# Attention inside a feed-forward kernel: the 144 keys of a pair of heads laid out key by key, as 128 and 16 rows

## The chip, the core and the metric

The kernel runs on one core of one Trainium2 chip. A core has TensorE (PE, with its weight loads shown as an engine of their own, PEld), VectorE (DVE), ScalarE (ACT), GpSimd (POOL) and the DMA queues, of which this kernel uses SyncE's (SP). The metric is the device time of one execution in microseconds; less is better. Each engine works through its own list of instructions in order and waits on semaphores for the others.

## What is computed

An attention over pooled keys and values, then two feed-forward layers:

```python
k_p = k.reshape(B, H, Sp, pool, D).mean(axis=3)      # B 8, H 8, S 576, D 64, pool 8, Sp 72
v_p = v.reshape(B, H, Sp, pool, D).mean(axis=3)
scores = scale * np.matmul(q, k_p.transpose(0, 1, 3, 2))
scores = scores - np.max(scores, axis=-1, keepdims=True)
attn = np.exp(scores)
attn = attn / (np.sum(attn, axis=-1, keepdims=True) + 1e-09)
out = np.matmul(attn, v_p)                            # then (4608 tokens, 512)
x = leaky(x @ w1_in) @ w1_out                         # 512 -> 2048 -> 512
x = (h * clip(h + 3, 0, 6) / 6) @ w2_out, h = x @ w2_in
```

All is float32. Where the kernel wants float32 accuracy at the rate of the shorter format, it splits an operand into a rounded part (`_hi`) and the rest (`_lo`) and adds three products: hi by hi, hi by lo, lo by hi.

## The kernel before

**Units and tiles.** The attention is cut into 32 units: 8 batches by 4 pairs of heads. A unit has 576 queries, 72 pooled keys for each of its two heads, and 64 columns of values for each. The feed-forward work is cut into 9 tiles of 512 tokens for each layer, 18 in all, each of 8 steps. The four units of batch 0 run ahead of everything; the 28 units of batches 1 to 7 are laid between the products of tiles 0 to 6, four units to a tile. That stretch is 45 to 735 us of the span; behind it only feed-forward work stands.

**What sets the order.** It is written by hand. A tile has 64 places (8 steps by 8), and `UNIT_PLACES` (line 49) says at which place of the tile each of the nine stages of each of its four units stands, on every engine alike: (0, 3, 4, 5, 6, 9, 11, 12, 14) for the first unit, and so on. TensorE's list is feed-forward products with a stage's products put in at its place. What an engine does at a place, it does there, late or not.

**The stages of a unit** (`stage`, once for each engine; ps_att is its two PSUM banks, 0 and 1):

- `place_k`: ACT puts the summed keys of both heads into `kT`, 144 columns, head 0 in 0 to 71 and head 1 in 72 to 143. `scores`: PE makes 5 products (L1910), one for each block of 128 queries. The blocks begin at 0, 128, 256 (half 0) and at 384, 448 (half 1), so that the last one shares 64 queries with the one before it. DVE takes the maxima (L1538) and subtracts them (L1543) for the two halves. `exp` is ACT's (L1193); `normalize` and `divide` are DVE's (L1549, L1553, L1557). `prob` then holds 10 rows of 72 for each query: block by block, head by head.
- `turn_p0`, `turn_p1`: PE turns the probabilities (L1928) so that keys stand on the partitions. A piece is one head of one block: 72 keys by 128 queries. Head 0 goes to bank 0, head 1 to bank 1. Half 0 has 6 whole pieces. Half 1 has 4, and those of the last block turn only its new 64 queries (`AGAIN`), that is 64 of its 128 rows. ACT rounds both heads at once into `pT_hi` (L1202), DVE subtracts for `pT_lo` (L1564).
- `pv0`, `pv1`: PE multiplies with the values, for each head the three products v_hi by pT_hi, v_hi by pT_lo, v_lo by pT_hi (L1729 to L1731): 72 rows, 384 queries in `pv0` and 192 in `pv1`, six products each. `v_hi[:, hd]` is zero but for its head's 64 columns, so that all six add into one bank. ACT copies the result (L1211).

**The values** come as 72 rows for each head; DVE sums them over the pool of 8 (`sum_v`, L1577), ACT rounds them (`round_v`, L1220), POOL subtracts (`v_lo`, L847). They go to their own places of the tile, some 7 places or more ahead of `pv0` in all tiles but tile 0.

**Batch 0** uses plain float32 values and probabilities (`v_f`, `pT_f`, L1942), two products where the others have six.

## Time and profile before

| | |
|---|---|
| median of 3 runs | 1659.18 us (1653.12 to 1662.17) |
| profiled execution | 1650.04 us, of which the span is 1648.2 us |
| PE busy, matmuls | 1636.8 us, 99%, 13947 instructions |
| PEld busy, weight loads | 1614.8 us, 98% |
| DVE, ACT, POOL busy | 68%, 41%, 26% |
| stretch with attention, 45 to 735 us | 5735 matmul records, PE busy 686.7 of 690 us |
| granted TensorE clock | 0.999 of 2.4 GHz |

Matmul records overlap: each lasts some 0.28 us from its first to its last cycle, while the next begins some 0.11 us after it. So what an instruction costs TensorE is read from the distance between the starts of two records, not from its length. A stage put between feed-forward products costs the distance from its first record to a product behind it, less what the products themselves take.

### The profile page before, as it was taken

Reading aid. Unit: us, or ns where it says so; the run is one execution under the profiler, and the core shown is the slowest. Engines: PE = TensorE matmul, PEld = TensorE weight load, DVE = VectorE, ACT = ScalarE, POOL = GpSimd, SP = SyncE. Lnnn points to the kernel's source line nnn. Section 1 sums busy time; section 2 is a strip of 40 time slices with the busy share of each in tenths; the row PEclk is TensorE's granted clock in tenths of the full one; section 3 lists DMA queues with packets and bytes.
Section 4 is the critical chain, followed back from the end, with each engine's and each line's share of the span. In section 5 each row is a group of like instructions: output and inputs, shape, how many; then the busy total and the mean of one; then the engine's idle time right before and its main releaser. Section 6 shows DMA issues by size and latency. Waiting matters only on the chain.

```text
span 1648.2 us, 40178 instructions
## 1 busy us (share of the span) xinstructions
PE 1636.8 (99%) x13947; PEld 1614.8 (98%) x13947; DVE 1120.2 (68%) x2159; ACT 676.4 (41%) x1427; POOL 429.3 (26%) x451
## 2 busy tenths in 40 slices
PE   9999999999999999999999999999999999999998
PEld 8999999999999999999999999999999999999998
DVE  6768777686776867756455666676767676766665
ACT  5554443333332433333233444444444444444443
POOL 4346552021120212103335572030211111111100
PEclk9999999999999999999999999999999999999999
DMA  7746878778686786867789998898989898989894
GB/s 222 259 140 221 284 254 261 225 216 277 201 268 219 231 267 201 272 193 262 260 254 358 312 358 302 297 337 296 341 297 336 282 339 294 336 288 340 294 323 156
DMA packets 228572, 447.94 MB, mean 272 GB/s; under 512 B 23872, under 2 KB 48448, under 8 KB 219200
## 3 DMA queue, kind: packets, MB, share of 16 engines
q1 hardware_dynamic: 228416, 445.74, 80.9%
q8 instruction: 113, 1.85, 0.4%
q14 instruction: 43, 0.35, 0.1%
HBM read 379.58 MB, written 66.06 MB: 270 GB/s over the span
## 4 chain that ended last, share of the span: by engine, by line
PE 81%; DVE 2%; issue 1%; DMA 1%; ACT 0%; POOL 0%; DVEq 0%; ACTq 0%
PE ps_h L1804 36%; PE ps_y L1750 31%; PE ps_y L1891 5%; PE ps_att L1891 4%; PE ps_att L1928 2%; PE ps_att L1910 2%; PE ps_att L1729 1%; PE ps_att L1731 1%; PE ps_att L1730 1%; DMA w_in_split<-stage 1%; POOL stage L934 0%; DVE prob L1557 0%; PE ps_att L1741 0%; DVE h L1458 0%; DVE gate L1392 0%
## 5 line engine op out<-in xcount | busy, mean ns | idle before, releaser
L1804 PE MATMUL ps_h<-xs_hi,ring 128*128 128x256 f32 x3808 | 796.0, 280 | 1.8 <-DVE h L1458 0.8
L1804 PEld LDWEIGHTS ps_h<-xs_hi,ring 128*128 128x128 f32 x3808 | 635.9, 188 | 6.8 <-issue 3.6
L1804 PE MATMUL ps_h<-xs_lo,ring 128*128 128x256 f32 x1904 | 528.1, 277 | 0.0
L1804 PEld LDWEIGHTS ps_h<-xs_lo,ring 128*128 128x128 f32 x1904 | 358.6, 188 | 0.0
L1138 ACT ACTIVATE g_hi<-gate 128x512 fp32r<-128x512 f32 x288 | 182.1, 632 | 380.2 <-DVE gate L1392 200.6
L1750 PE MATMUL ps_y<-g_hi,wout_hi 128*128 128x256 f32 x1152 | 320.2, 278 | 0.6 <-DVE y_stage L1454 0.6
L1750 PE MATMUL ps_y<-g_hi,wout_lo 128*128 128x256 f32 x1152 | 319.2, 277 | 0.0
L1750 PE MATMUL ps_y<-g_lo,wout_hi 128*128 128x256 f32 x1152 | 319.1, 277 | 0.0
L1750 PEld LDWEIGHTS ps_y<-g_hi,wout_hi 128*128 128x128 f32 x1152 | 216.3, 188 | 1.2 <-DVE y_stage L1454 1.0
L1750 PEld LDWEIGHTS ps_y<-g_lo,wout_hi 128*128 128x128 f32 x1152 | 217.1, 188 | 0.0
L1750 PEld LDWEIGHTS ps_y<-g_hi,wout_lo 128*128 128x128 f32 x1152 | 216.3, 188 | 0.0
L1458 DVE TENSOR_TENSOR u<-ps_h,p 128x256 f32<-128x256 f32 x272 | 114.1, 419 | 124.0 <-PE ps_h L1804 104.7
L1127 ACT ACTIVATE pre<-h,three 128x512 f32<-128x512 f32 x144 | 103.2, 716 | 206.2 <-DVE h L1458 179.7
L1750 PE MATMUL ps_y<-wout_hi,g_hi 128*128 128x256 f32 x640 | 177.1, 277 | 0.0
L1750 PE MATMUL ps_y<-wout_lo,g_hi 128*128 128x256 f32 x640 | 177.1, 277 | 0.0
L1750 PE MATMUL ps_y<-wout_hi,g_lo 128*128 128x256 f32 x640 | 177.1, 277 | 0.0
L1398 DVE SCALAR_TENSOR_TENSOR gate<-pre,h 128x512 f32<-128x512 f32 x144 | 107.1, 744 | 67.2 <-ACT pre L1127 67.2
L1458 DVE TENSOR_TENSOR h<-ps_h,u 128x256 f32<-128x256 f32 x272 | 113.7, 418 | 54.6 <-PE ps_h L1804 53.0
L1407 DVE TENSOR_TENSOR g_lo<-gate,g_hi 128x512 fp32r<-128x512 f32 x144 | 109.8, 763 | 56.8 <-ACT g_hi L1138 56.6
L1411 DVE SCALAR_TENSOR_TENSOR g_lo<-gate,g_hi 128x512 fp32r<-128x512 f32 x144 | 105.6, 734 | 35.0 <-ACT g_hi L1138 34.9
L913 POOL TENSOR_TENSOR xs_lo<-x_stage,xs_hi 128x512 fp32r<-128x512 f32 x20 | 28.7, 1434 | 386.7 <-ACT xs_hi L1107 386.7
L1750 PEld LDWEIGHTS ps_y<-wout_lo,g_hi 128*128 128x128 f32 x640 | 120.3, 188 | 0.0
(155 smaller groups left out, 2862.1 us busy)
## 6 DMA issues: line engine op xcount, KB each, us to landing
ring<-w_in_split SPq DMA_DIRECT2D x920, 256.0 KB, 4.0
w_sums<-w_out_sums SPq DMA_DIRECT2D x64, 1024.0 KB, 6.2
w_in_split<-ring SPq DMA_DIRECT2D x56, 256.0 KB, 3.7
w_in_split<-stage SPq DMA_DIRECT2D x56, 256.0 KB, 3.9
k_raw<-in_kT SPq DMA_DIRECT2D x32, 288.0 KB, 4.0
q_raw<-in_qT SPq DMA_DIRECT2D x32, 288.0 KB, 5.3
v_raw<-in_v SPq DMA_DIRECT2D x32, 288.0 KB
x0T<-x_stage SPq DMA_DIRECT2D x32, 288.0 KB, 4.2
```

Of the source, the lines that this page charges most:

```text
L913: nc.gpsimd.tensor_tensor(xs_lo[second][:, r], x_block(r), xs_hi[second][:, r].bitcast(F32), ALU.subtract).then_inc(x_ready, 1 if r < NT4 ...
L1127: nc.scalar.activation(pre[:, upper], h[:, upper], ACT.Relu, bias=three[:]).then_inc(pre_ready, 1)
L1138: nc.scalar.activation(g_hi[layer == 2][:, g_slot(i, upper)], gate[:, upper], ACT.Copy, scale=1.0 / 6.0 if layer == 2 else 1.0).then_inc(g ...
L1398: nc.vector.scalar_tensor_tensor(gate[:, upper], pre[:, upper], 6.0, h[:, upper], ALU.min, ALU.mult).then_inc(gate_ready, 1)
L1407: nc.vector.tensor_tensor(g_lo[0][:, slot], gate[:, upper], g_hi[0][:, slot].bitcast(F32), ALU.subtract).then_inc(g_ready, 1)
L1411: nc.vector.scalar_tensor_tensor(g_lo[1][:, slot], gate[:, upper], 1.0 / 6.0, g_hi[1][:, slot].bitcast(F32), ALU.mult, ALU.subtract).then_ ...
L1458: return nc.vector.tensor_tensor(to, banks[bank], other, ALU.add)
L1750: mm = pe.matmul(bank[:, cols], left[a], right[b][:, cols], start=first and half == 0 and n == 0, stop=last and n == 2, skip_group_check=True)
L1804: mm = pe.matmul(banks[BANK_OF[r]], a, b[:, r, c, :], start=r in OPENS and c == 0 and n == 0, stop=c == 1 and n == 2, skip_group_check=True)
L1891: mm = pe.matmul(pair_banks[r], left[a], right[b], start=i == 0 and n == 0 and r in PAIR_OPENS, stop=i == HF - 1 and n == 2, skip_group_ch ...
L1910: mm = pe.matmul(u.ps[:, half, at * PAIR_KEYS:(at + 1) * PAIR_KEYS], q_of(b, c)[:, begins:begins + P], u.kT[:], start=True, stop=True)
L1928: mm = pe.transpose(at.ps[0:KEYS, hd, to:to + P - rows.start], u.prob[rows, SLOTS[half].start + 2 * j + hd, :], ident[rows, rows])
```

## The change

The 144 scores of a block stand key by key: key 0 of head 0, key 0 of head 1, key 1 of head 0. Keys 0 to 63 of both heads are then 128 adjacent columns, and keys 64 to 71 are 16.

- `place_k` writes every other column of `kT`. The maxima, sums, subtraction and division read and write `prob` as block, key, head (a step of two elements between the keys of one head).
- `turn_p0`, `turn_p1`: for each block one piece of 128 keys and one of 16, over all 128 queries; the last block, too, is turned whole. The 16-row pieces of half `half` go to bank `half` and come first, the 128-row pieces to the other bank. Batch 0 keeps 72-row pieces, one for each head, and turns its last block whole.
- ACT makes three copies for each half: the 16 rows and the 128 rows of `pT_hi`, and once more the 16 rows to partitions 64 to 79. DVE makes two subtractions: that of the 16 rows goes to partitions 32 to 47 of the same buffer, that of the 128 rows to `pT_lo`.
- `pv0`, `pv1`: four products: v_hi by p_hi, v_lo by p_hi (128 rows), one over 80 rows that does all three products of the last 16 rows at once (its weights hold v_hi, v_hi and v_lo at partitions 0, 32 and 64), and v_hi by p_lo (128 rows). They wait separately for what each needs.
- The values are loaded as 128 rows, and as 96 rows that repeat the last 16 six times, 256 KB and 192 KB instead of 288 KB, in two DMAs. `sum_v` sums 128 partitions and then multiplies by a mask (`v_masked`, new), which clears the other head's columns. `round_v` is one instruction of 256 columns, `v_lo` one of 128 rows and one of 16. The mask is made once by DVE (`make_mask`), and POOL clears `pT_hi` once when the products of batch 0 are done.

The tables of places are unchanged. In the built program the turns of 16 rows name a tile of 128 by 32 of the array, all others 128 by 128; before, the turns of 64 queries named 64 by 128, all others 128 by 128.

The diff, cut to its core:

```diff
...
+FULL = 64
+REST = 2 * (KEYS - FULL)
+REST_LO = slice(32, 32 + REST)
+AGAIN = slice(64, 64 + REST)
+VALUE_COPIES = 6
+VALUE_ROWS = VALUE_COPIES * REST
...
-                sp.dma_start(buffers(b, c).v_raw[:], v[b, c]).then_inc(v_loaded[c], 16)
+                to = buffers(b, c).v_raw
+                if first(b):
+                    sp.dma_start(to[0:KEYS], v_first[c]).then_inc(v_loaded[c], 16)
+                else:
+                    sp.dma_start(to[:, 0], v_full[b - 1, c]).then_inc(v_loaded[c], 16)
+                    sp.dma_start(to[0:VALUE_ROWS, 1], v_rest[b - 1, c]).then_inc(v_loaded[c], 16)
...
+            pool.wait_ge(pv_done, 2 * PAIRS)
+            pool.memset(units[0].pT_hi[0:AGAIN.stop].bitcast(F32), 0.0).then_inc(pT_zeroed, 1)
             blocks_lo(2)
             v_lo(1, 0)
...
+                        for rows, bank in ((slice(0, REST), half), (slice(0, P), 1 - half)):
+                            nc.scalar.activation(u.pT_hi[rows, bank, 0:n_q], u.ps[rows, bank, 0:n_q],
+                                                 ACT.Copy).then_inc(pT_hi_ready, 1)
+                        act.wait_ge(pT_hi_ready, 3 * (2 * n + half) + 1)
+                        nc.scalar.activation(u.pT_hi[AGAIN, half, 0:n_q],
+                                             u.pT_hi[0:REST, half, 0:n_q].bitcast(F32), ACT.Copy
+                                             ).then_inc(pT_hi_ready, 1)
...
-                for hd in range(2):
-                    nc.scalar.activation(u.v_hi[:, hd, hd * D:(hd + 1) * D], u.v_sum[:, hd, :],
-                                         ACT.Copy).then_inc(v_hi_ready, 1)
+                nc.scalar.activation(u.v_hi[:], u.v_masked[:].rearrange("p s h d -> p s (h d)"),
+                                     ACT.Copy).then_inc(v_hi_ready, 1)
...
-                    nc.vector.tensor_tensor(u.pT_lo[:, :, 0:n_q], u.ps[0:KEYS, :, 0:n_q],
-                                            u.pT_hi[:, :, 0:n_q].bitcast(F32), ALU.subtract
-                                            ).then_inc(pT_ready, 1)
+                    for k, (to, rows, bank) in enumerate((
+                            (u.pT_hi[REST_LO, half], slice(0, REST), half),
+                            (u.pT_lo, slice(0, P), 1 - half))):
+                        dve.wait_ge(pT_hi_ready, 3 * (2 * n + half) + k + 1)
+                        nc.vector.tensor_tensor(to[:, 0:n_q], u.ps[rows, bank, 0:n_q],
+                                                u.pT_hi[rows, bank, 0:n_q].bitcast(F32),
+                                                ALU.subtract).then_inc(pT_ready, 1)
...
+                dve.wait_ge(v_summed, n + 1)
+                nc.vector.tensor_tensor(u.v_masked[:],
+                                        u.v_sum[:].unsqueeze(2).to_broadcast([P, 2, 2, D]),
+                                        u.v_mask[:].unsqueeze(3).to_broadcast([P, 2, 2, D]),
+                                        ALU.mult).then_inc(v_masked, 1)
...
-                            rows = slice(AGAIN if begins == S - P else 0, P)
-                            to = begins + rows.start - PART_BEGINS[half]
-                            mm = pe.transpose(
-                                at.ps[0:KEYS, hd, to:to + P - rows.start],
-                                u.prob[rows, SLOTS[half].start + 2 * j + hd, :],
-                                ident[rows, rows])
+                            to = begins - PART_BEGINS[half]
+                            row = u.prob[:, BLOCKS_AT[half].start + j]
+                            if first(b):
+                                rows, keys = KEYS, row[:, :, bank]
+                            else:
+                                part = slice(FULL, KEYS) if bank == half else slice(0, FULL)
+                                rows, keys = ((P, REST)[bank == half],
+                                              row[:, part].rearrange("p k h -> p (k h)"))
+                            mm = pe.transpose(at.ps[0:rows, bank, to:to + P], keys, ident[:])
...
-                        pe.wait_ge(pT_ready, 2 * n + half + 1)
-                        for hd in range(2):
-                            mm = product(u.ps[:, half, 0:n_q],
-                                         (u.v_hi[:, hd, :], u.v_lo[:, hd, :]),
-                                         (u.pT_hi[:, hd, 0:n_q], u.pT_lo[:, hd, 0:n_q]),
-                                         hd == 0, hd == 1)
+                        acc, p_hi = u.ps[:, half, 0:n_q], u.pT_hi[:, 1 - half, 0:n_q]
+                        pe.wait_ge(pT_hi_ready, 3 * (2 * n + half) + 2)
+                        pe.wait_ge(pT_ready, 2 * (2 * n + half) + 1)
+                        pe.matmul(acc, u.v_hi[:, 0], p_hi, start=True, stop=False)
+                        pe.matmul(acc, u.v_lo[:], p_hi, start=False, stop=False)
+
+                        pe.wait_ge(pT_hi_ready, 3 * (2 * n + half) + 3)
+                        pe.matmul(acc, u.v_hi[0:AGAIN.stop, 1], u.pT_hi[0:AGAIN.stop, half, 0:n_q],
+                                  start=False, stop=False)
+                        pe.wait_ge(pT_ready, 2 * (2 * n + half) + 2)
+                        mm = pe.matmul(acc, u.v_hi[:, 0], u.pT_lo[:, 0:n_q], start=False, stop=True)
```

**TensorE's list**, before, at the second turn of a unit and with its neighbours (L1804 and L1750 are feed-forward products; the shape is that of the result):

```order
L1750 MATMUL ps_y<-g_hi,wout_lo 128x256
L1928 MATMUL ps_att<-ident,prob 72x128
L1928 MATMUL ps_att<-ident,prob 72x64
L1928 MATMUL ps_att<-ident,prob 72x128
L1928 MATMUL ps_att<-ident,prob 72x64
L1804 MATMUL ps_h<-xs_hi,ring 128x256
L1804 MATMUL ps_h<-xs_lo,ring 128x256
```

The same place after (L1829 and L1883 are the feed-forward products now):

```order
L1829 MATMUL ps_y<-g_hi,wout_lo 128x256
L2013 MATMUL ps_att<-ident,prob 16x128 x2
L2013 MATMUL ps_att<-ident,prob 128x128 x2
L1883 MATMUL ps_h<-xs_hi,ring 128x256
L1883 MATMUL ps_h<-xs_lo,ring 128x256
```

Two short and two long turns took the place of an alternation of whole and half blocks; nothing else moved. The first turn has six pieces of 72 rows before, and three of 16 and three of 128 after.

**VectorE's list**, before, from the second subtraction of one unit to the sum of the next unit's values:

```order
L1564 TENSOR_TENSOR pT_lo<-ps_att,pT_hi 72x2x192
L1458 TENSOR_TENSOR u<-ps_h,p 128x256
L1458 TENSOR_TENSOR h<-ps_h,u 128x256
L1458 TENSOR_TENSOR h<-ps_h,p 128x256
L1392 SCALAR_TENSOR_TENSOR gate<-h 128x512
L1571 TENSOR_REDUCE k_sum<-k_raw 128x72
L1458 TENSOR_TENSOR h<-ps_h,u 128x256
L1577 TENSOR_REDUCE v_sum<-v_raw 72x128
L1407 TENSOR_TENSOR g_lo<-gate,g_hi 128x512
```

The same place after:

```order
L1620 TENSOR_TENSOR pT_hi<-ps_att,pT_hi 16x192
L1620 TENSOR_TENSOR pT_lo<-ps_att,pT_hi 128x192
L1506 TENSOR_TENSOR u<-ps_h,p 128x256
L1506 TENSOR_TENSOR h<-ps_h,u 128x256
L1506 TENSOR_TENSOR h<-ps_h,p 128x256
L1440 SCALAR_TENSOR_TENSOR gate<-h 128x512
L1627 TENSOR_REDUCE k_sum<-k_raw 128x72
L1506 TENSOR_TENSOR h<-ps_h,u 128x256
L1648 TENSOR_REDUCE v_sum<-v_raw 128x128
L1651 TENSOR_TENSOR v_masked<-v_sum,v_mask 128x256
L1455 TENSOR_TENSOR g_lo<-gate,g_hi 128x512
```

One subtraction became two, and the multiplication by the mask stands between the sum of the values and the subtraction for g_lo.

**ScalarE's list** in tile 0, around the first turn of the first unit of batch 1, before:

```order
L1138 ACTIVATE g_hi<-gate 128x512
L1202 ACTIVATE pT_hi<-ps_att 72x768
L1220 ACTIVATE v_hi<-v_sum 72x64 x2
L1254 ACTIVATE h<-ps_h 128x512
L1188 ACTIVATE kT<-k_sum 64x72 x2
```

And after:

```order
L1175 ACTIVATE g_hi<-gate 128x512
L1247 ACTIVATE pT_hi<-ps_att 16x384
L1247 ACTIVATE pT_hi<-ps_att 128x384
L1250 ACTIVATE pT_hi<-pT_hi 16x384
L1268 ACTIVATE v_hi<-v_masked 128x256
L1302 ACTIVATE h<-ps_h 128x512
L1225 ACTIVATE kT<-k_sum 64x72 x2
```

Three copies stand where one stood, ahead of the rounding of the values.

## Rows read from the trace of the kernel before

**Rows 1.** The page's head and its engines: busy time, share, instructions.
```profile
span 1648.2 us, 40178 instructions
...
PE 1636.8 (99%) x13947; PEld 1614.8 (98%) x13947; DVE 1120.2 (68%) x2159; ACT 676.4 (41%) x1427; POOL 429.3 (26%) x451
```
**Rows 2.** Waits of PE from 45 to 735 us: total us, times, longest.
```profile
PE ps_att L1729 <- POOL v_lo L847: 1.2, 1, 1.2
...
PE ps_att L1729 <- DVE pT_lo L1564: 0.6, 3, 0.2
```
**Rows 3.** Timeline of PE, a first turn: start us, length us, instruction, count.
```profile
398.11 0.81 PE L1928 MATMUL ps_att<-ident,prob 128*72 128x128 f32 x6
...
398.88 0.28 PE L1804 MATMUL ps_h<-xs_lo,ring 128*128 128x256 f32 x1
```
**Rows 4.** Timeline of PE, the second turn of the same unit.
```profile
404.05 0.86 PE L1928 MATMUL ps_att<-ident,prob 128*72 128x128 f32 x4
...
405.06 0.28 PE L1804 MATMUL ps_h<-xs_lo,ring 128*128 128x256 f32 x1
```
**Rows 5.** Timeline of PEld: weight loads of the second turn, then of the first.
```profile
404.25 0.52 PEld L1928 LDWEIGHTS ps_att<-ident,prob 64*72 64x72 f32 x3 [0.18 <-issue]
...
398.01 0.65 PEld L1928 LDWEIGHTS ps_att<-ident,prob 128*72 128x72 f32 x6
```
**Rows 6.** Timeline of PE, first and last records of pv0, then of pv1.
```profile
401.59 0.34 PE L1729 MATMUL ps_att<-pT_hi,v_hi 72*128 72x384 f32 x1
...
402.47 0.34 PE L1731 MATMUL ps_att<-pT_hi,v_lo 72*128 72x384 f32 x1
...
406.99 0.25 PE L1729 MATMUL ps_att<-pT_hi,v_hi 72*128 72x192 f32 x1
...
407.53 0.27 PE L1731 MATMUL ps_att<-pT_hi,v_lo 72*128 72x192 f32 x1
```
**Rows 7.** Timeline around a late pv0: PE, and ACT's copy ahead of it.
```profile
462.25 0.28 PE L1750 MATMUL ps_y<-g_hi,wout_lo 128*128 128x256 f32 x1
462.70 0.41 PE L1729 MATMUL ps_att<-pT_hi,v_hi 72*128 72x384 f32 x1 [0.17 <-DVE pT_lo L1564]
...
460.76 0.80 ACT L1202 ACTIVATE pT_hi<-ps_att 72x768 fp32r<-72x768 f32 x1
```
**Rows 8.** Groups by line and shape: busy us, mean ns, idle before.
```profile
L1202 ACT ACTIVATE pT_hi<-ps_att 72x384 fp32r<-72x384 f32 x28 | 13.5, 481 | 16.1 <-PE ps_att L1928 16.1
L1211 ACT ACTIVATE x_stage<-ps_att 128x192 f32<-128x192 f32 x30 | 9.9, 332 | 49.4 <-PE ps_att L1731 48.8 <-PE ps_att L1942 0.6
L1564 DVE TENSOR_TENSOR pT_lo<-ps_att,pT_hi 72x384 fp32r<-72x384 f32 x28 | 15.4, 550 | 14.4 <-ACT pT_hi L1202 14.4
L1470 DVE TENSOR_TENSOR gs<-gate 128x128 f32<-128x128 f32 x64 | 18.6, 291 | 2.0
L1538 DVE TENSOR_REDUCE row_max<-ps_att 128x6 f32<-128x432 f32 x29 | 17.6, 607 | 33.5 <-PE ps_att L1910 33.5
```
**Rows 9.** Timeline of DVE around a sum of values with work behind it.
```profile
488.07 1.21 DVE L1577 TENSOR_REDUCE v_sum<-v_raw 72x128 f32<-72x1024 f32 x1
...
490.54 0.42 DVE L1458 TENSOR_TENSOR h<-ps_h,u 128x256 f32<-128x256 f32 x1 [0.93 <-PE ps_h L1804]
```
**Rows 10.** Timeline of DVE and PE: a unit's division and its first turn.
```profile
415.30 1.70 DVE L1557 TENSOR_TENSOR prob<-prob,row_inv 128x432 f32<-128x432 f32 x2
...
417.47 0.38 PE L1928 MATMUL ps_att<-ident,prob 128*72 128x128 f32 x2
```
**Rows 11.** Timeline of POOL and PE: the first unit of batch 1.
```profile
53.83 2.58 POOL L847 TENSOR_TENSOR v_lo<-v_sum,v_hi 72x64 fp32r<-72x64 f32 x2 [2.28 <-ACT v_hi L1220]
...
56.47 0.45 PE L1729 MATMUL ps_att<-pT_hi,v_hi 72*128 72x384 f32 x1 [1.22 <-POOL v_lo L847]
```
**Rows 12.** Two stretches of 60 us without attention: matmul records, granted clock, DMA share, GB/s.
```profile
1260.00:1320.00 60.00, 60.00 (x512) 1.00 0.89 307
1320.00:1380.00 60.00, 60.00 (x532) 1.00 0.94 327
```

144 lines of the change are left out of this document (93 added, 51 removed).

## The prediction

> **What bounds the kernel now.** I read the page's engines first: TensorE's matmuls are busy 99% of the span, its weight loads 98%, no other engine above 68% [rows 1]. Then its waits in the stretch with attention: about 3 us in 690, the longest 1.2 us for POOL's v_lo, three short ones for pT_lo [rows 2]. So the time is the sum of the distances between TensorE's records, and the change is worth what it does to them, unless it makes a new wait. The timeline gives each stage's price as the distance from its first record to the second feed-forward product behind it, less one product (0.12 us). A first turn: 398.11 to 398.88 is 0.77, less 0.12 is 0.65 us for six records, 0.109 each [rows 3]. A second turn has only four, two of them half as wide, and costs more: 404.05 to 405.06 is 1.01, less 0.12 is 0.89 us [rows 4]. The weight loads say why: in the first turn six stand in 0.65 us, each under the matmul before it; in the second the load of the second piece begins only at 404.25, 0.20 us after the first matmul's start, and three take 0.52 us [rows 4, 5]. A record whose rows change from 128 to 64, or back, does not overlap its neighbour. pv0: five distances from 401.59 to 402.47, 0.176 us a product; pv1: 406.99 to 407.53, 0.108 us a product [rows 6].
>
> **Part by part.** There are 28 units in batches 1 to 7.
>
> 1. *Products with values.* Six become four in each of pv0 and pv1: 2 x 0.176 + 2 x 0.108 = 0.57 us less for a unit. That 128 or 80 rows stand where 72 stood costs nothing by the row of the neighbours: going from 128-row products to 72-row ones adds nothing visible in [rows 6]. 80 rows is no half tile either; the instruction names 128 by 128.
>
> 2. *What a change of the tile costs.* By pace alone the old second turn would take two whole records and two half ones, 2 x 0.109 + 2 x 0.055 = 0.33 us. It takes 0.89, so 0.56 us lies in four changes (in, out, in, out): 0.14 us each [rows 4, 5]. The new turns have no 64-row piece, but their 16-column pieces name a tile of 128 by 32. No row shows a change of columns. Bounds: 0 (only the change of rows is shown to cost), and 0.14, the nearest row. I take 0.14, since what the loads show is that a load does not slip under a matmul of another tile, and that need not know rows from columns. Each new turn has two changes, in and out. The Trainium skill, TensorEngine Tiling (Array Packing), Key Properties, says that a change of the tiling mode drains TensorE; the row on the 64-row pieces agrees, for columns nothing here shows it. By the rule the sum is the one I take, without it some 16 us more would be gained.
>
> 3. *Turns.* First turn: 0.65 + 2 x 0.14 = 0.93, or 0.28 us more. Second: four records at 0.109 are 0.65 - 0.22 = 0.43, plus 0.28 is 0.71, or 0.18 us less. Together 0.10 us more for a unit. A weight load of 128 columns instead of 72 stays under a 0.109 us record, as the 128-column loads of the 0.108 us products of pv1 do [rows 6].
>
> One unit: 0.10 - 0.57 = -0.47 us; 28 units: -13.2 us.
>
> 4. *The way from the turn to pv.* Before, one copy and one subtraction of 768 columns stand in a row ahead of the first product: in a late unit 460.76 to 462.70, 1.94 us, 0.80 of them the copy's [rows 7]. After, ACT copies 384 columns three times at 0.48 us and DVE subtracts 384 columns twice at 0.55 us [rows 8]; the first product needs the second copy (0.96) and the first subtraction (0.48 + 0.55 = 1.03), the last the second subtraction (0.96 + 0.55 = 1.5), the third product the third copy (1.45). So pv0 can start some 0.8 us earlier after its turn. In the first unit of a tile TensorE now waits there, 462.25 to 462.70 for a product of 0.12, 0.33 us [rows 7]; three such waits are counted [rows 2], with the slow record behind each about 0.4 us. They go: -1.2 us. For half 1 the three copies take 3 x 0.33 and the first product needs 0.66 + 0 us against 0.48 + 0.55 before [rows 8]: no new wait.
>
> 5. *ACT.* Per unit 3 x 0.48 - 0.80 and 3 x 0.33 - 0.48, about +1.1 us, less 0.1 for round_v; 28 us on an engine busy 41% [rows 1]. What is queued behind the copies is a rounding of g or a copy out of ps_h; ACT idles 16 us before the second copies alone [rows 8]. Taken at nothing; if that cover is gone, it is up to 0.6 us at each of 56 turns.
>
> 6. *DVE.* Two subtractions of half the width for one: +0.15 us twice. The mask: 256 columns, between 0.29 us (128 columns) and 0.55 (384) [rows 8], so 0.42, plus its wait for the sum: 0.5 us. Behind it stands an addition to u or the subtraction for g_lo; where an addition follows, DVE idles 0.93 us just after it [rows 9]. Hidden, bounds 0 and 0.5 us a unit.
>
> 7. *Tile 0.* There the chain of values is late: POOL's v_lo runs 53.83 to 56.41 and TensorE waits 1.22 us for it [rows 11]. The mask (0.5) and ACT's three copies ahead of the rounding (0.65) lie on it: +1.0 us once.
>
> 8. *Batch 0.* Its four second turns lose their four tile changes and gain nothing new: 4 x (0.89 - 0.43) = 1.8 us, of which I count half, since this stretch waits for other engines: -0.9 us. POOL's clearing of pT_hi and the making of the mask stand where both engines idle.
>
> 9. *DMA.* 448 KB for 288 a unit, one more issue on SP's queue, 4.5 MB in all. No wait of TensorE in the stretch is for a transfer [rows 2]. Nothing.
>
> 10. *Pace of the products behind.* Feed-forward products run at 0.117 or 0.113 us, at the same granted clock: 512 against 532 records in 60 us [rows 12]. After a first turn the slower pace holds until pv0, after a second the faster. Which the new turns leave behind I can't tell: some 20 products x 28 x 0.0045 us, 2.5 us either way; taken at zero.
>
> Sum: -13.2 - 1.2 + 1.0 - 0.9 = -14.3 us, from 1650.04 to 1635.7 us for the profiled execution. The median shown is 9 us above that execution, within 1653 to 1662; paces as in point 10, which move by 3 us for each tile, are enough for that. Carried to the median: 1659.2 - 14.3 = 1644.9 us.
>
> **Rivals.**
>
> *A: a change of columns is free.* For it: only rows are shown to cost. Against: the loads. 28 x 4 x 0.14 = 15.7 us more gained: 1629 us.
>
> *B: the 16-column turns take two passes.* The scores, plain float32, leave two records for each product, the turns one. If the narrow tile loses what lets a turn go in one pass, 5 x 28 records cost 0.11 us more each: +15.4, or 1660 us, no change. Nothing in the trace speaks for or against. The Trainium skill, TensorEngine Tiling (Array Packing), Restrictions, says that column tiling disables the transpose mode for float32 input; that would do it. No run here shows it yet.
>
> *C: strided reads on VectorE.* Maxima and sums now step over two elements. If such a reduction takes twice its 0.61 and 0.45 us [rows 8], in both stages, division ends 2.1 us later. In the fourth unit of a tile it ends 417.00 and the turn starts 417.47 [rows 10]: 0.5 us of slack, in the other units 0.5 to 2. Some 2.6 us of wait a tile, 18 us: 1663 us.
>
> *D, slower: the 16-column turns take two passes and overlap nothing.* The nearest row is the second turn's: a record without overlap is 0.2 us [rows 4, 5], two are 0.4 instead of 0.109, so 140 x 0.29 = +41 us: 1686 us. It decides against the change from 0.16 us more for each 16-column turn. Against: pieces of one tile follow each other, so that only the first should drain.
>
> *That the change doesn't do what it says:* the list shows four products and whole turns; excluded.
>
> **Numbers.** Half a percent, about what a measurement of this kernel can tell from no change, is 8.3 us. Forecast 0.50, A 0.18, B 0.13, C 0.07, D 0.08, the rest 0.04. Predicted is the forecast's 1645 us. The range reaches from A to B and C: 1628 to 1663 us. Faster: A and 0.43 of the forecast's 0.50 (its bounds, 4 us for points 5, 6 and 10, leave a little beyond the limit), 0.61; same: the rest of the forecast, B and most of C, 0.26; slower: D and its neighbours, 0.13.
>
> **What would show it.** In the profile after: matmul records fewer by 4 x 28 = 112; pv0 and pv1 of four records, 0.70 and 0.44 us; a first turn near 0.93 us and a second near 0.71 by the same reading as above. With 0.65 and 0.43 it is A. With two records for each 16-column turn it is B, with one every 0.2 us D. Row_max at 1.2 us is C, and then PE waits for DVE's prob at the turns. The wait for pT_lo should be gone and that for v_lo near 55 us longer. I am wrong if the waits of PE grow by more than 3 us or the products elsewhere change their pace.

## The result

The kernel after takes 1642.29 us (median of 17 runs, 1631.2 to 1652.65) against 1653.12 us for the kernel before, run beside it (17 runs, 1647.63 to 1662.17). The ratio is 0.993, 95% interval 0.991 to 0.994: 11 to 12 us faster, where I had forecast 14.3. The profiled execution took 1635.86 us with a span of 1634.0, 14.2 us under the span of before.

The number came out, and by luck: two terms of the sum were wrong, and their errors cancel. The attention saved twice what I had summed, and about half of that was lost again in the stretch behind it, in which the change touched nothing. Most of what follows is on that second part.

The page of after, head and engines. Beside [rows 1]: 112 matmul records fewer, as the prediction named; ScalarE +30 us, VectorE +27 us of busy time:

```profile
span 1634.0 us, 40399 instructions
...
PE 1612.2 (99%) x13835; PEld 1596.6 (98%) x13835; DVE 1147.5 (70%) x2246; ACT 706.7 (43%) x1511; POOL 427.3 (26%) x451
```

Timeline of PE after, one unit: first turn, pv0, second turn, pv1, each with a product behind it (start us, length us, instruction, count; a line that joins records shows the shape of the first):

```profile
383.98 0.82 PE L2013 MATMUL ps_att<-ident,prob 128*16 128x128 f32 x6
384.55 0.37 PE L1883 MATMUL ps_h<-xs_hi,ring 128*128 128x256 f32 x1
384.76 0.28 PE L1883 MATMUL ps_h<-xs_lo,ring 128*128 128x256 f32 x1
...
387.37 0.33 PE L2031 MATMUL ps_att<-pT_hi,v_hi 128*128 128x384 f32 x1
...
387.89 0.34 PE L2038 MATMUL ps_att<-pT_lo,v_hi 128*128 128x384 f32 x1
...
389.45 0.60 PE L2013 MATMUL ps_att<-ident,prob 128*16 128x128 f32 x4
389.80 0.37 PE L1883 MATMUL ps_h<-xs_hi,ring 128*128 128x256 f32 x1
390.01 0.28 PE L1883 MATMUL ps_h<-xs_lo,ring 128*128 128x256 f32 x1
...
391.94 0.25 PE L2031 MATMUL ps_att<-pT_hi,v_hi 128*128 128x192 f32 x1
...
392.25 0.27 PE L2038 MATMUL ps_att<-pT_lo,v_hi 128*128 128x192 f32 x1
```

By the reading of [rows 3, 4] (first record to the second product, less 0.12) the first turn costs 384.76 - 383.98 - 0.12 = 0.66 us, before 0.65; the second 390.01 - 389.45 - 0.12 = 0.44 us, before 0.89. I had put 0.93 and 0.71. pv0 is four records 0.173 us apart, pv1 four 0.103 us apart, about as forecast. Rival A had named 0.65 and 0.43.

Weight loads of that second turn:

```profile
389.36 0.45 PEld L2013 LDWEIGHTS ps_att<-ident,prob 128*16 128x16 f32 x4
```

Four loads in 0.45 us, among them the step from 16 to 128 columns, where three took 0.52 in [rows 5]: each slips under the matmul before it.

Waits of PE after, first from 45 to 721 us (the stretch with attention), then from 745 us to the end (us in total, times, longest):

```profile
PE ps_h L1883 <- ACT p L1343: 2.1, 2, 1.3
PE ps_att L2031 <- DVE pT_hi L1620: 1.2, 2, 0.7
PE ps_y L1829 <- DVE y_stage L1502: 0.6, 1, 0.6
PE ps_att L2031 <- POOL v_hi L880: 0.5, 1, 0.5
```
```profile
PE ps_h L1883 <- DVE u L1506: 5.5, 5, 2.4
PE ps_h L1883 <- ACT p L1343: 1.1, 2, 0.5
PE ps_h L1883 <- DVE h L1506: 1.0, 4, 0.3
PE ps_h L1883 <- ACT h L1351: 0.3, 1, 0.3
```

Those of [rows 2] are gone or smaller; in their place stand two for the subtraction of pT_hi, in tile 0. The wait for p behind a second turn is new, and so is the one for u in the stretch without attention, where the kernel before had only 0.7 us for p and 0.2 for h. Over the whole span PE's waits add up to 16.3 us, against 6.7 before. The prediction had named a growth of more than 3 us as a sign that it is wrong; it grew by 9.6. I cut the span at the starts of tiles (each has 336 products of the line that is L1804 before and L1883 after; a start is the first of them):

| us | before | after | difference |
|---|---|---|---|
| start to the end of the attention (first product of the eighth tile) | 747.6 | 720.8 | -26.8 |
| from there to the end | 900.6 | 913.2 | +12.6 |
| of this, the last seven tiles | 572.5 | 583.4 | +10.9 |

Timeline of DVE and PE around one of the new waits:

```profile
1375.95 0.93 DVE L1459 SCALAR_TENSOR_TENSOR g_lo<-gate,g_hi 128x512 fp32r<-128x512 f32 x1 [0.44 <-ACT g_hi L1175]
1381.67 0.42 DVE L1506 TENSOR_TENSOR u<-ps_h,p 128x256 f32<-128x256 f32 x1 [4.79 <-issue]
...
1382.24 0.36 PE L1883 MATMUL ps_h<-xs_hi,ring 128*128 128x256 f32 x1 [2.45 <-DVE u L1506]
```

VectorE does nothing for 4.79 us and waits for no engine and no transfer ("issue"). Of the last seven tiles the first six are a loop in VectorE's list (`Fori(PAIR_TILE + 1, ALL_TILES - 1)`, 318 instructions a turn with waits and register work), and such a gap, 2.7 to 4.8 us, stands behind each of the five jumps that close a turn. What came in over the DMA queues from 1160 to 1530 us, before and then after (queue, kind: packets, MB, share):

```profile
q1 hardware_dynamic: 48331, 117.11, 90.7%
q8 instruction: 26, 0.43, 0.4%
```
```profile
q1 hardware_dynamic: 46432, 112.86, 88.3%
q8 instruction: 26, 0.43, 0.4%
q14 instruction: 21, 0.17, 0.1%
```

After, one queue brings 21 packets of code, 8 KB each; before, none. I took a block as 128 instructions; the runs with the head at 60 and at 80, below, bear it out, since three blocks then hold 378 instructions from the start of one and not 398. In the built program the loop's head stands 83 instructions later than before (its own 318 are the same; the trace's records of VectorE, counted between the closing jumps and up to them, say the same): the masks, the second subtractions and their waits are ahead of it. From the times of the fetches against the instructions that VectorE has reached, its place in a block of 128 was about slot 4 before and is about slot 87 now. 4 + 318 ends in the third block, 87 + 318 in the fourth.

How the 12.6 us lie in PE's list: I took the distance between the starts of every two records behind the attention (7821 of them in both kernels) and what each has above 0.113 us. The distances over 0.12 us, that is waits and the slow records around them, hold 4.2 us before and 16.0 after; 13.3 of the 16.0 lie in the loop, where before has 1.8. The rest is the pace: many products follow each other at 0.117 instead of 0.113 us, at the same granted clock. That is 5.7 us before and 6.3 after, so next to nothing of the difference. But it is no constant: the fourteen profiles of this case have 4.4 to 14.8 us of it, with gaps in the loop or without. A time of the tail holds both, so I give the long distances beside it.

### The profile page after: what moved, and what is told of

Same layout as the page of the kernel before. It is cut to its first block, busy times and chain, and to the rows that moved or that the text cites. A ratio compares the mean times of both kernels' runs of the same rounds, so it can differ in the third digit from the quotient of the medians.

```text
span 1634.0 us, 40399 instructions
## 1 busy us (share of the span) xinstructions
PE 1612.2 (99%) x13835; PEld 1596.6 (98%) x13835; DVE 1147.5 (70%) x2246; ACT 706.7 (43%) x1511; POOL 427.3 (26%) x451
## 4 chain that ended last, share of the span: by engine, by line
PE 76%; issue 3%; DVE 2%; DMA 1%; ACT 1%; SPq 0%; DVEq 0%; POOL 0%; ACTq 0%
PE ps_h L1883 35%; PE ps_y L1829 29%; PE ps_y L1970 5%; PE ps_att L1970 4%; PE ps_att L1989 1%; PE ps_att L2013 1%; DMA w_in_split<-stage 1%; DVE h L1506 1%; DVE gate L1446 1%; ACT pre L1164 1%; PE ps_att L2031 0%; PE ps_att L2038 0%; PE ps_att L2032 0%; PE ps_att L2035 0%; DMA x0T<-x_stage 0%
## 5 line engine op out<-in xcount | busy, mean ns | idle before, releaser
L1883 PE MATMUL ps_h<-xs_hi,ring 128*128 128x256 f32 x3808 | 798.2, 280 | 11.3 <-DVE u L1506 5.5
L1883 PEld LDWEIGHTS ps_h<-xs_hi,ring 128*128 128x128 f32 x3808 | 636.7, 188 | 19.3 <-issue 17.4
L1883 PE MATMUL ps_h<-xs_lo,ring 128*128 128x256 f32 x1904 | 528.7, 278 | 0.0
L1883 PEld LDWEIGHTS ps_h<-xs_lo,ring 128*128 128x128 f32 x1904 | 358.2, 188 | 0.0
L1829 PE MATMUL ps_y<-g_hi,wout_hi 128*128 128x256 f32 x1152 | 320.3, 278 | 0.6 <-DVE y_stage L1502 0.6
L1829 PE MATMUL ps_y<-g_hi,wout_lo 128*128 128x256 f32 x1152 | 319.4, 277 | 0.0
L1829 PE MATMUL ps_y<-g_lo,wout_hi 128*128 128x256 f32 x1152 | 319.4, 277 | 0.0
L1829 PEld LDWEIGHTS ps_y<-g_hi,wout_hi 128*128 128x128 f32 x1152 | 216.5, 188 | 0.9 <-DVE y_stage L1502 0.8
L1829 PEld LDWEIGHTS ps_y<-g_hi,wout_lo 128*128 128x128 f32 x1152 | 216.8, 188 | 0.0
L1829 PEld LDWEIGHTS ps_y<-g_lo,wout_hi 128*128 128x128 f32 x1152 | 216.7, 188 | 0.0
L1829 PE MATMUL ps_y<-wout_lo,g_hi 128*128 128x256 f32 x640 | 177.3, 277 | 0.0
L1829 PE MATMUL ps_y<-wout_hi,g_hi 128*128 128x256 f32 x640 | 177.3, 277 | 0.0
L1829 PE MATMUL ps_y<-wout_hi,g_lo 128*128 128x256 f32 x640 | 177.3, 277 | 0.0
L1829 PEld LDWEIGHTS ps_y<-wout_hi,g_hi 128*128 128x128 f32 x640 | 120.4, 188 | 0.0
```

What stands on the lines that cost most here:

```text
L1829: mm = pe.matmul(bank[:, cols], left[a], right[b][:, cols], start=first and half == 0 and n == 0, stop=last and n == 2, skip_group_check=True)
L1883: mm = pe.matmul(banks[BANK_OF[r]], a, b[:, r, c, :], start=r in OPENS and c == 0 and n == 0, stop=c == 1 and n == 2, skip_group_check=True)
```

## Experiments

Ratios are to the kernel before on the same chip; half a percent is 8 us.

### The loop's place in the code

Three kernels made from after and one from before set the head of that loop, and nothing else. The diff (the slot is 0, 60, 80, and 100 in the kernel before):

```diff
-            with dve.Fori(PAIR_TILE + 1, ALL_TILES - 1) as T:
+            only = OrderedEngineSet([dve.engine])
+            with dve.bass.Fori(PAIR_TILE + 1, ALL_TILES - 1, 1, engines=only,
+                               head_slot={dve.engine: 0}) as T:
```

> The kernel after, with one thing changed: the first instruction of VectorE's last loop (tiles 11 to 17, 318 instructions a turn) is put at the start of a block of code. What has to be explained: the 883 us behind the attention take 12.6 us more after the change (913.2 against 900.6), though nothing in them was changed. Theory 1, place of the loop: the instructions added ahead of it moved the loop's head from about slot 4 of a block of 128 to about slot 87, so that its body lies in four blocks of 8 KB instead of three, and the jump back finds its first block gone. In the trace after, code is fetched 25 times between 1140 and 1560 us (8 KB each), before not once, and VectorE is idle 2.7 to 4.8 us just behind five of its six jumps. By it this kernel has no fetches there, the tail takes about 901 us and the ratio to before is 0.985 (1628 us), against 0.993 for after. Theory 2, chance or buffers: the waits come from the execution or from where buffers now lie, and the head does not matter: 25 fetches, tail 913 us, ratio 0.993.

(Two slips in it: the 883 us are the 900.6 and 913.2 of the table, and the loop runs over tiles 11 to 16.) Measured: 0.9887 (0.986 to 0.992), tail 906.3 us with 8.7 us of long distances, six fetches after 1100 us, none between 1126 and 1547.

> The kernel after with the head of VectorE's last loop at slot 60: 60 + 318 = 378 instructions end inside the third block of 128. Theory 1 (place of the loop): as with the head at 0, no fetches between 1140 and 1560 us, tail about 901 us, ratio 0.985. If blocks were of another size than 128, or if it were the distance from the start of a block that counts, some of the loss would show. Theory 2: 913 us, 0.993.

Measured: 0.9862 (0.983 to 0.989), tail 906.8 us with 7.7 us of long distances, no fetch between 1129 and 1543.

> The kernel after with the head at slot 80, 20 further than in the run with 60: 80 + 318 = 398 reaches into a fourth block of 128. Theory 1: 20 slots bring the whole loss back: some 25 fetches between 1140 and 1560 us, VectorE idle 2.5 to 5 us behind a jump, tail about 913 us, ratio 0.993. Theory 2: the same as the run with 60, whatever that is.

Measured: 0.9959 (0.994 to 0.998), tail 929.4 us, worse than forecast: 24.9 us of long distances (the gaps behind its five jumps are 3.9 to 4.6 us, and one of 3.4 stands at the loop's entry) and 13.7 of slow pace. Behind two waits of PE, of 2.4 and 2.2 us, which end at 1146 and 1317 us, the granted clock also stands at 0.50, the level of 1.2 GHz, for some microseconds.

> The kernel before, with the head of VectorE's last loop at slot 100; nothing of the attention is changed. Theory 1: 100 + 318 lies in four blocks, so the old kernel gets the loss of the new one: fetches between 1140 and 1560 us, waits of TensorE of 1 to 2.5 us at the starts of five or six tiles, tail 913 us instead of 901, ratio 1.007. Theory 2 (it takes the new attention's buffers or its timing): ratio 1.000, tail 901 us.

Measured: 1.0083 (1.006 to 1.011), tail 919.3 us with 13.7 us of long distances. Code queue and waits of PE from 1160 to 1530 us, of the kernel after with the head at 80 and then of the kernel before with it at 100:

```profile
q14 instruction: 21, 0.17, 0.2%
...
PE ps_h L1886 <- DVE u L1507: 7.7, 4, 2.2
```
```profile
q14 instruction: 23, 0.19, 0.2%
...
PE ps_h L1807 <- DVE u L1459: 4.8, 5, 1.4
```

With the head at 60 the same stretch has no such queue and 0.2 us of waits. Twenty slots, from 60 to 80, are worth 1 percent, 16 us, in a kernel whose work is the same to the last instruction, and the old kernel gets the loss of the new one when its loop is put badly. Theory 2 is out. The Trainium skill, Runtime: NRT & Kernel Launch, Instruction fetch mechanics, says that an engine other than TensorE holds 32 KiB of code, and that a taken branch to code outside it waits for a fetch. The runs agree (three blocks of the body and one fetched ahead are 32 KB); it gives blocks of 16 KiB, the packets here are 8 KB.

The runs with 0 and 60 lose something at one place: at the first turn of the loop, VectorE idles 3.6 us and PE waits 1.3 to 1.4 us. The head was put there by a jump over padding. So I moved it without one:

```diff
+            EXTRA_AT = (3, 7)
...
+                    if m in EXTRA_AT and isinstance(T, int) and ATT_TILES <= T <= PAIR_TILE:
+                        dve.wait_ge(eps_ready, PAIRS)
```

> The kernel after, with 63 waits of VectorE more, each on a semaphore long at its value, two in each of the 32 steps between its two loops. They compute nothing; they move the head of its last loop from slot 87 to slot 22 of a block, and the loop is entered from the instruction ahead of it, not by a jump over padding. By the place of the loop: no code fetched between 1140 and 1530 us, no wait of 2 us at the first turn of the loop (which the runs with a set head had, VectorE idle 3.6 us), tail 901 to 904 us, ratio 0.984 to 0.986. If instructions of VectorE cost what they take, 63 more can only be slower than the kernel after: 0.993 or more.

Measured: 0.9848 (0.982 to 0.987), median 1628.26 us against 1653.99. No wait of PE at all from 1160 to 1530 us. The tail, 905.6, is a little above the forecast; its long distances are down to 4.3 us, as in the kernel before, and what is left above 901 is pace (10.5 us for 5.7). 63 more instructions on VectorE make the kernel 13 us faster. Measured again later: 0.9843 (0.982 to 0.987), tail 906.1 us with 4.5 us of long distances (label a_waits_2, below).

```diff
-            with dve.Fori(PAIR_TILE + 1, ALL_TILES - 1) as T:
+            only = OrderedEngineSet([dve.engine])
+            with dve.bass.Fori(PAIR_TILE + 1, ALL_TILES - 1, 1, engines=only, hint_back_edge=True) as T:
```

> The kernel after, with the head of VectorE's last loop left at slot 87 and a branch hint armed at the top of each turn (one instruction), which names the target of the jump that closes the loop. The body still lies in four blocks, so code must still be fetched, 20 times or more between 1140 and 1560 us. If the cost is that the first block is asked for only when the jump is taken, VectorE's idle time behind it goes from 2.7 to 4.8 us to under 1 us and the ratio is 0.985. If the cost is the traffic of the fetches or their number, it stays 0.993.

Measured: 0.990 (0.986 to 0.994), tail 903.4 us with 7.7 us of long distances. Half a miss: the gaps behind the jumps are gone, as by the first case, but so are the fetches (none between 1122 and 1534 us), though the body still reaches into a fourth block. One reading is that without the hint it is the block behind the loop, fetched ahead in vain, that drives the first one out; no run here tests it. One new gap appears, in VectorE's list of the last tile, for which PE waits 1.7 us:

```profile
1576.72 0.42 DVE L1507 TENSOR_TENSOR u<-ps_h,p 128x256 f32<-128x256 f32 x1 [4.13 <-issue]
```

It stands 40 us behind the end of the loop (the last closing jump, not taken, is at 1532.3), and a packet of code comes in during it. No other profile has a gap over 2 us there, so I put it down to the hint; why it comes so late, the runs don't say. Its profiled span, 1625.9 us, is as short as that of the run with the waits; its four timed runs spread from 1627.9 to 1640.6, so it can't be ranked against it.

### A change of columns, a change of rows

```diff
-                    for bank in ((0, 1), (1, 0))[half]:
-                        if half == 1 and bank == 0 and at is u:
-                            pe.wait_ge(x0_copied, 2 * n + 1)
-                        for j, begins in enumerate(BLOCK_AT[half]):
+                    if half == 1 and at is u:
+                        pe.wait_ge(x0_copied, 2 * n + 1)
+                    for j, begins in enumerate(BLOCK_AT[half]):
+                        for bank in ((0, 1), (1, 0))[half]:
```

> The kernel after, with the pieces of a turn in another order: 16 keys and 128 keys of one block, then of the next, where all of 16 columns came first. The instructions are the same. A first turn now changes its tile six times instead of two, a second four times instead of two: 6 more changes in a unit, 168 in all. By the step of my prediction (0.14 us a change, rows or columns alike) the first turn goes from 0.66 to 1.22 us, the second from 0.44 to 0.72, +23.5 us, ratio 1.007. By the rival (a change of columns is free, as the first look at after suggests) both stay at 0.66 and 0.44 us and the ratio stays 0.993.

Measured: 0.9935 (0.991 to 0.996). Its two turns, with the product from which the reading ends:

```profile
382.87 0.82 PE L2013 MATMUL ps_att<-ident,prob 128*16 128x128 f32 x6
...
383.65 0.28 PE L1883 MATMUL ps_h<-xs_lo,ring 128*128 128x256 f32 x1
...
388.34 0.60 PE L2013 MATMUL ps_att<-ident,prob 128*16 128x128 f32 x4
...
388.90 0.28 PE L1883 MATMUL ps_h<-xs_lo,ring 128*128 128x256 f32 x1
```

0.78 and 0.56 us, less 0.12: 0.66 and 0.44, to the hundredth what they are with all narrow pieces first. 168 more changes of columns cost nothing.

```diff
-                            rows = slice(AGAIN if begins == S - P else 0, P)
+                            rows = slice(0, P)
```

> The kernel before, with the last block of queries turned whole (128 rows instead of the 64 new ones), and nothing else: one part of the change alone. By the price of a change of rows (0.14 us, four in each second turn) the second turn goes from 0.88 to 0.44 us though it turns more; 28 units x 0.45 us and four of batch 0: -12.5 to -14 us, ratio 0.992. VectorE's list is not touched, so its loop stays in three blocks and the tail at 901 us. If the slowness were of the half pieces themselves and not of the change between tiles, the two records would still be long: then the first half of this gain only.

Measured: 0.9919 (0.989 to 0.995). The second turn of the kernel before, whole:

```profile
395.03 0.60 PE L1928 MATMUL ps_att<-ident,prob 128*72 128x128 f32 x4
395.38 0.37 PE L1804 MATMUL ps_h<-xs_hi,ring 128*128 128x256 f32 x1
395.59 0.28 PE L1804 MATMUL ps_h<-xs_lo,ring 128*128 128x256 f32 x1
```

0.56 - 0.12 = 0.44 us for four whole pieces, against 0.89 for two whole and two half ones. One line of the diff holds 0.45 x 28 = 12.6 us: as much as the whole change shows in the end. So the price of my point 2 is one of rows. That it lies in the change between 64 and 128 rows, and not in the half pieces alone, the records of [rows 4] show one by one: they start at 404.05, 404.25, 404.43 and 404.67, the next product at 404.84. The two whole pieces take 0.20 and 0.23 us there until the half piece behind them starts, where whole pieces among themselves take 0.109. How much of the 0.18 us of a half piece is the change back, no run shows, since no two half pieces follow each other. So a change costs 0.11 us if a half piece by itself takes what a whole one does (0.45 / 4), and my 0.14 if it takes half.

### The new wait for p

In all profiles of the new form PE waits behind some second turns for ScalarE's copy p: 2.1 us after, 5.1 in the run with alternating pieces, 3.0 in the one with 63 waits, 4.7 with the head at 60. ScalarE's rows at one of them, after (the wait for p ends 566.74):

```profile
560.00 0.85 ACT L1247 ACTIVATE pT_hi<-ps_att 16x384 fp32r<-16x384 f32 x2 [3.51 <-PE ps_att L2013]
560.88 0.52 ACT L1250 ACTIVATE pT_hi<-pT_hi 16x384 fp32r<-16x384 f32 x1
...
565.91 0.42 ACT L1120 ACTIVATE stage<-s_sum 128x256 fp32r<-128x256 f32 x1 [1.37 <-DMA w_in_split<-stage]
566.23 0.36 ACT L1343 ACTIVATE p<-ps_h 128x256 f32<-128x256 f32 x1
```

The same place before:

```profile
580.77 0.81 ACT L1202 ACTIVATE pT_hi<-ps_att 72x768 fp32r<-72x768 f32 x1 [3.51 <-PE ps_att L1928]
...
585.74 0.42 ACT L1083 ACTIVATE stage<-s_sum 128x256 fp32r<-128x256 f32 x1
586.06 0.37 ACT L1295 ACTIVATE p<-ps_h 128x256 f32<-128x256 f32 x1
```

From the first copy to p it is 5.29 us before, 6.23 after, and what lies between is a wait for a store to free `stage`. At the same time PE comes 0.8 us sooner (0.36 of pv0, 0.45 of the second turn). Before, p is ready at 586.43 and the product that needs it starts at 587.33: 0.9 us of slack, less 0.8, less 0.94, is about the 0.84 us for which PE waits after. The kernel before with its block turned whole, 0.45 us shorter there, has no such wait, though ScalarE waits 2.7 us there for the store, in all, where the kernel before waits 0.7; the kernel before with its loop at slot 100 has 2.6. So a part of the late stores comes without the new bytes and the new copies. Three runs asked which of the causes can be taken away.

Late copy (the third copy of the first half moved to the place before pv0):

```diff
-                        act.wait_ge(pT_hi_ready, 3 * (2 * n + half) + 1)
-                        nc.scalar.activation(u.pT_hi[AGAIN, half, 0:n_q],
-                                             u.pT_hi[0:REST, half, 0:n_q].bitcast(F32), ACT.Copy
-                                             ).then_inc(pT_hi_ready, 1)
+                        if half == 1:
+                            copy_again(b, c, half)
...
+                for name, c in stages_at(T, place + 1):
+                    if name == "pv0":
+                        copy_again(T + 1, c, 0)
```

> The kernel of the run with 63 more waits, and ScalarE's third copy of the first half (16 rows, 384 columns, 0.52 us) not right behind the other two, but one place ahead of pv0. What it should tell: in every profile of the new form TensorE waits behind the second turn of the first or second unit of tiles 2 to 6 for ScalarE's copy p, 3.0 to 5.1 us in all and up to 1.8 us at once, which the kernel before does not. Theory 1, ScalarE's list: the third copy of the first turn puts off the four roundings for the next layer's weights behind it, with them the store that frees their buffer (ScalarE waits 0.7 to 1.4 us for it), and so the copy p. Then these waits fall from 3 to 5 us to under 2, the second turns' mean from 0.61 to about 0.48 us, ratio 0.982 to 0.983 against 0.985. Theory 2, the transfers: the stores are late because the values now come in two transfers and with more bytes, or because all runs faster. Then the place of the copy changes nothing: 3 to 5 us, 0.985.

> The kernel with 63 more waits again, on the same chip as the run with the late copy, to compare the two and to see how far its time and the waits for p repeat: 0.983 to 0.987, waits for p 3 to 5 us.

Measured: late copy 0.9849 (0.983 to 0.987), kernel with 63 waits 0.9843 (0.982 to 0.987). No gain: waits for p 2.4 us against 1.4 in its twin, ScalarE's for the store 5.8 against 3.5, and 2.1 us more for the late copy itself. Theory 1 had named under 2 us and gets no support. The expected 3 to 5 us of the twin was too narrow: from profile to profile the same kernel shows 1.4 and 3.0, so one profile of each can't tell a microsecond. (The kernel after, too, has only 2.1 us, less than the 3.0 to 5.1 that the expectation gives for every profile.)

Fewer bytes:

```diff
-                    sp.dma_start(to[0:VALUE_ROWS, 1], v_rest[b - 1, c]).then_inc(v_loaded[c], 16)
+                    sp.dma_start(to[0:1, 1], v_rest[b - 1, c, 0:1]).then_inc(v_loaded[c], 16)
```

> The kernel with 63 more waits; of the last 16 rows of the values one row is loaded instead of 96 for each unit, so it leaves out most of the values of keys 64 to 71 (the work of every engine is the same). The transfer of the second part shrinks from 192 KB to 2 KB, a unit's values from 448 to 258 KB (288 in the kernel before). The late copy of ScalarE left TensorE's waits for p where they were (2.4 us in three, and 1.6 us of ScalarE's wait at once for the store of the next layer's weights), and the store lands 4.5 to 4.6 us after its issue where it took 3.7 before. Theory 2, the bytes: with them gone the store lands within 3.9 us, ScalarE waits for it under 2 us in all instead of 3.5 to 5.8, TensorE for p under 1 us instead of 1.4 to 5.1, second turns' mean 0.48 us. Theory 3, the shorter attention: the products are fewer, so TensorE comes 1 us sooner to the place where it needs p, and the store simply has less time: then nothing changes, 3 to 5 us.

Measured: 0.9854 (0.983 to 0.988); waits for p 1.9 us, ScalarE's for the store 4.1; the first store of a tile lands in 3.4 to 4.6 us. Between the two theories, and within the 1.4 to 3.0 us that the same kernel shows with all its bytes: the bytes are not the cause, or not alone.

Load moved:

```diff
+                if place == loads[1] - 6 and not is_first(T):
+                    load_v(T + 1, 2)
                 for c in range(PAIRS):
                     if place == loads[c]:
-                        if c < PAIRS - 1:
+                        if c == 1 and not is_first(T):
+                            load_k_q(T + 1, c + 1)
+                        elif c < PAIRS - 1:
                             load_unit(T + 1, c + 1)
```

> The kernel with 63 more waits; the values of the third unit are loaded 6 places (9 us) sooner, from tile 1 on, so that their 448 KB do not stand ahead of the stores of the next layer's weights. Theory 2: the same bytes, but the stores land sooner (under 4 us), and the waits for p go below 1.5 us: ratio 0.982 to 0.983. Theory 3: no change, 0.985.

Measured: 1.0065 (1.004 to 1.009), 35 us slower than the kernel it was made from. It tells nothing of the theories, since the move made a wait of its own. Waits of SP's queue and of PE from 136 to 757 us:

```profile
SPq L532 <- DVE v_sum L1652: 55.8, 11, 9.9
...
PE ps_h L1891 <- ACT p L1347: 23.6, 6, 5.5
```

`load_v` waits until the sum of the unit before has been made, and that sum stands at place 13; at place 9 the issue holds SP's queue for it, and behind it stand the streams and stores of weights. In the kernel that it was made from the same wait is 4.7 us in all. I had read that the queue was free, not what the issue waits for.

The waits of PE are only two thirds of the 35 us. In or right behind each of its six long waits (1.6 to 5.5 us) the granted clock falls to 0.50, the level of 1.2 GHz, for 30.6 us in all; in the run with 63 waits it stays at 1.00 until the last microseconds. A stretch behind such a wait and the one after it (length, PE busy and records, granted clock, DMA share, GB/s):

```profile
177.30:180.50 3.20, 3.20 (x17) 0.50 0.88 270
181.00:186.00 5.00, 5.00 (x45) 1.00 0.96 334
```

Products start 0.21 us apart there instead of 0.11, so the 30.6 us cost some 14 us (an estimate from these rows).

## Why the prediction came out

Point by point, in the prediction's numbers; us are for the 28 units where nothing else is said.

- **1, products**: -0.57 a unit forecast, -0.59 measured (medians 1.06 to 0.70, 0.67 to 0.45). Right, and that 128 or 80 rows cost what 72 did.
- **2, a change of the tile**: the step that failed. I took 0.14 us for a change of columns because it was the nearest row; it is 0 to the hundredth (after, and the run with alternating pieces). 28 x 4 x 0.14 = 15.7 us, rival A. The 0.14 itself rests on half pieces that take half the time of whole ones; without that it is 0.11. The Trainium skill, TensorEngine Tiling (Array Packing), Key Properties, has a change of tiling mode drain the engine; that holds here for rows, 64 against 128, and not for columns, 32 against 128. I gave that rival 0.18 with one argument against it, the loads of [rows 5], which speak of rows alone: with 0 and 0.14 as the only bounds and no row between, it deserved near half.
- **3, turns**: +0.10 a unit forecast, -0.44 measured, all of it through point 2. No second record appears for a narrow turn (B and D are out): 140 records of the 16-column form and 140 of the 128-column form in the trace, as many as there are pieces.
- **4, waits for pT_lo**: gone in pv0 as said.
- **5, ACT at nothing**: mis-sized. Its own copies are as forecast (0.47, 0.46 and 0.52 us); the cover was not complete: p has 0.9 us of slack in the second unit of a tile, and a later store and the shorter stages eat it up. That the new copies make the store late, the run with the late copy does not bear out. With all waits and what they leave in the records the second turns cost 3.3 us more than their median in after.
- **6, DVE at nothing**: held but for tile 0, where the sum of values and the mask (0.43 us, forecast 0.42) stand ahead of a subtraction: PE waits there at 62 and 98 us, 1.2 us.
- **7, tile 0's v_lo**: +1.0 forecast, -1.1 measured (pv0 at 55 us costs 1.46 us with its wait, before 2.54). ScalarE is indeed later by 0.7 us after its turn, but POOL's two instructions take 54.63 - 53.64 = 0.99 us where they took 2.58. I had read the 2.58 of [rows 11] as what two of them take. By the view of POOL's line, before and then after (shortest, median and longest in ns), it is one instruction of 2.30 us among 56 with a median of 0.32:

```profile
L847 POOL TENSOR_TENSOR v_lo<-v_sum,v_hi x56: 314/320/2302, 53.8 to 718.1; 72x64 fp32r<-72x64 f32 x56
```
```profile
L880 POOL TENSOR_TENSOR v_lo<-v_masked,v_hi x28: 452/458/910, 53.6 to 692.3; 128x128 fp32r<-128x128 f32 x28
L880 POOL TENSOR_TENSOR v_hi<-v_masked,v_hi x28: 447/455/788, 54.2 to 692.8; 16x128 fp32r<-16x128 f32 x28
```

  The three profiles of the old form all have one such instruction at this place (2.30, 2.30 and 2.16 us), the eleven of the new form none. What makes it long stays open.
- **8, batch 0**: the first turn of batch 1 begins 0.8 us sooner (50.06 for 50.89), forecast 0.9.
- **9, DMA at nothing**: open. The stores that free `stage` land later in most profiles of the new form (3.5 to 5.5 us; 3.3 to 3.9 in the kernel before, 3.3 to 4.4 in it with the whole block), but taking the new bytes away did not settle it.
- **C, strided reads**: out. Row_max takes 0.606 us, before 0.607, with its step of two elements; the two divisions of a unit take 1.58 us together, before 1.63.
- **The place of the loop**: no step of mine at all, and here the prediction was saved. I had taken the stretch without attention as unchanged because its instructions are. 12.6 us went there: 7.0 us are PE's waits (7.9 against 0.9), 4.8 the slow records around them, 0.6 the pace. In the five profiles with the 63 waits the long distances are 4.3 to 5.2 us instead of 16.0. With the loop put right in any of the ways tried the tail takes 902 to 907 us instead of 913.
- **10, pace**: taken at zero, and 0.6 us between the two profiles behind the attention. The 4.4 to 14.8 us over all profiles say that this is luck too.

In sums: -29.1 for the stages at their medians (1.04 a unit, read from the record ahead of a stage to the second product behind it), +3.0 for waits within them, -0.8 for batch 0 and 0.1 that I can't assign give the -26.8 of the table, and +12.6 behind it the -14.2 of the span. My -14.3 was two errors of about 12.5 us with different signs: too little gain by that in the attention (15.7 from point 2, less what the waits took back), and no loss at all for the loop. That they cancel is luck; the median of the runs, 11 to 12 us faster, came out with them. The version that beats both kernels is the change with the loop's head moved by 63 waits: 1628.3 and 1627.0 us in two sets of runs, ratio 0.985 and 0.984.

Three things stay open: what sets the pace of 0.113 or 0.117 us at the same granted clock (up to 10 us from profile to profile), how the late stores share between more bytes and less time (2 to 5 us), and what makes one instruction of POOL long in the old form (1 us).

## To carry to other kernels

An instruction added ahead of a loop is work in the loop's place too: count the body in blocks of code, before and after the change, and look whether the code queue of the page has new packets; if it has, moving the loop by a few dozen idle instructions can be worth more than the change. Of two prices that the trace can't tell apart, don't take the nearest row as the likeliest. An issue that is moved forward in a queue brings its wait with it: read what it waits for and what stands behind. A length taken from one row is not yet a price: look at the shortest and the median of its group first. And a number that comes out proves no sum: the signs that a prediction names beside it (here the waits of PE) say whether the mechanism did.

## What the runs showed of the hardware

- Code for VectorE comes in blocks of 8 KB, and a loop of 318 instructions runs without a fetch with its head at slot 0, 22 or 60 of 128 (22 and 87 are reckoned, the others set); with it at 80, 87 or 100 there are 21 to 23 fetches in 370 us and gaps of 2.6 to 4.8 us at the jumps.
- Entering the loop by a jump cost one gap of 3.4 to 3.6 us; with a hint for the closing jump all gaps in the loop were gone, and one of 4.1 us stood 40 us behind its end.
- Turns of 16 columns (tile 128 by 32) between turns of 128 columns: 0.108 us each, loads hidden, no cost of the change. Turns of 64 rows between turns of 128: 0.45 us for four changes, 0.11 us a change or 0.14, by what a half piece is held to take.
- POOL takes 0.46 us for 128 by 128 elements (median of 28), 0.46 for 16 by 128, and took 0.32 for 72 by 64 (median of 56): three and a half times the elements for less than half more time.
- In or right behind waits of PE of 1.6 to 5.5 us the granted clock stood at 0.50 for 30.6 us in all in the run with the moved load, and products started 0.21 us apart instead of 0.11. Behind waits of up to 2.4 us in the loop it did so twice in the run with the head at 80, and not in after.
